# Tile sizes, first-tile attention, attend product, PSUM layout and engine loops of a chunked-attention and two-FFN kernel

## What is computed

```python
# q, k, v: (4, 8, 768, 64); mem_k, mem_v: (4, 8, 8, 64)
for c in range(768 // 32):               # chunks of 32 queries
    keys = [8 memory keys, 16 left, 32 own, 8 right]   # clipped at both ends
    scores = q_c @ keys.T / sqrt(64)
    a = exp(scores - max); a = a / (sum(a) + 1e-9)
    out[c] = a @ values
x  = out as (3072 tokens, 512)
x2 = (s * relu(x @ w_in1)**2 + b) @ w_out1           # 512 -> 2048 -> 512
h  = x2 @ w_in2;  result = (h * sigmoid(1.702 * h)) @ w_out2
```

## Time and profile before

| | us |
|---|---|
| median of 3 runs | 1269.33 |
| lowest and highest | 1268.78, 1270.19 |
| span of the profiled execution | 1269.2 |
| PE busy | 1252.3 |
| DVE, ACT, POOL busy | 655.9, 552.9, 96.9 |

### The profile page before, as it was taken

How to read it: one execution, slowest core, us unless ns; L and a number is a source line. 1 busy time by engine, 2 the same in 40 slices (tenths; PEclk the granted TensorE clock), 3 DMA queues, 4 the chain that set the end, 5 groups by cost and what they waited for, 6 DMA issues and landing times.

```text
span 1269.2 us, 20951 instructions
## 1 busy us (share of the span) xinstructions
PE 1252.3 (99%) x7168; PEld 1142.9 (90%) x7168; DVE 655.9 (52%) x2111; ACT 552.9 (44%) x1676; POOL 96.9 (8%) x78
## 2 busy tenths in 40 slices
PE   7999999999999999999999999999999999999998
PEld 5699999998999999999999999999999999999997
DVE  7788766666666666666645532333333332333322
ACT  7767555554555555555535532322222222222222
POOL 2255000000000000000005710000000000000000
PEclk9999999999999999999999999999999999999999
DMA  6545211212121212112013410000000101010000
GB/s 123 129 106 131 66 29 32 63 24 49 49 47 24 71 24 63 33 27 68 10 58 117 133 59 25 25 26 26 25 25 0 50 0 50 0 50 0 5 20 25
DMA packets 119555, 59.91 MB, mean 47 GB/s; under 512 B 93863, under 2 KB 110247, under 8 KB 119463
## 3 DMA queue, kind: packets, MB, share of 16 engines
q1 hardware_dynamic: 119463, 58.74, 17.6%
HBM read 46.14 MB, written 12.58 MB: 46 GB/s over the span
## 4 chain that ended last, share of the span: by engine, by line
PE 97%; DVE 2%; ACT 1%; issue 1%; DMA 0%; SPq 0%
PE psum L448 43%; PE psum L466 21%; PE psum L463 21%; PE psum L415 5%; PE psum L431 3%; PE psum L401 2%; PE psum L391 1%; PE psum L390 1%; DVE qk_lo L640 1%; ACT qk_hi L504 1%; DVE probs_n L671 0%; DVE masked L654 0%; DMA kv_raw<-in_mem_k_dram 0%; DVE x_lo L680 0%; DVE total_e L662 0%
## 5 line engine op out<-in xcount | busy, mean ns | idle before, releaser
L448 PE MATMUL psum<-x_hi,win_hi 128*128 128x384 f32 x1024 | 355.2, 347 | 0.0
L448 PE MATMUL psum<-x_hi,win_lo 128*128 128x384 f32 x1024 | 345.7, 338 | 0.0
L448 PE MATMUL psum<-x_lo,win_hi 128*128 128x384 f32 x1024 | 344.9, 337 | 0.0
L448 PEld LDWEIGHTS psum<-x_lo,win_hi 128*128 128x128 f32 x1024 | 193.2, 189 | 5.5
L448 PEld LDWEIGHTS psum<-x_hi,win_hi 128*128 128x128 f32 x1024 | 192.8, 188 | 5.6
L448 PEld LDWEIGHTS psum<-x_hi,win_lo 128*128 128x128 f32 x1024 | 192.7, 188 | 0.0
L466 PE MATMUL psum<-g_hi,wout_hi 128*128 128x384 f32 x512 | 171.6, 335 | 0.0
L466 PE MATMUL psum<-g_lo,wout_hi 128*128 128x384 f32 x512 | 171.5, 335 | 0.0
L466 PE MATMUL psum<-g_hi,wout_lo 128*128 128x384 f32 x512 | 171.3, 335 | 0.0
L640 DVE TENSOR_TENSOR qk_lo<-psum,qk_hi 64x128 fp32r<-64x128 f32 (+1 forms) x384 | 94.9, 275 | 128.0 <-ACT qk_hi L504 125.9
L539 ACT ACTIVATE g_hi<-gated 128x384 fp32r<-128x384 f32 x128 | 67.2, 525 | 196.5 <-PE psum L463 195.9
(11 more groups left out here) (61 smaller groups left out, 1585.6 us busy)
## 6 DMA issues: line engine op xcount, KB each, us to landing
w_raw<-in_moe_w_in_dram SPq DMA_DIRECT2D x32, 256.0 KB, 2.8
w_raw<-in_moe_w_out_dram SPq DMA_DIRECT2D x32, 256.0 KB, 2.8
kv_raw<-in_v_dram SPq DMA_DIRECT2D x32, 240.0 KB
kv_raw<-in_k_dram SPq DMA_DIRECT2D x31, 240.0 KB
x_scratch<-result SPq DMA_DIRECT2D x8, 768.0 KB, 3.3
kv_raw<-x_scratch SPq DMA_DIRECT2D x8, 768.0 KB, 4.3
q_raw<-in_q_dram SPq DMA_DIRECT2D x31, 192.0 KB
out_dram<-result SPq DMA_DIRECT2D x7, 768.0 KB, 3.6
```

Source lines behind the costliest of these rows:

```text
L448: last = nc.tensor.matmul(dst, w[:, f, kt, :], x[:, slot, kt, :], start=(i == 0), stop=(i == len(terms) - 1))
```

## The change

1. Part 0 is cut into tiles of 288, 288, 384, 384, 384, 384, 480 and 480 tokens; part 1 stays at 8 times 384.
2. Only 12 units (the first 288 tokens) come ahead of the first product, in 6 rounds of four heads each, with their own buffers and banks (`first_*` functions). Here the scores are 64-row products of 128 columns, POOL normalizes, and DVE copies the transposed probabilities. Three more rounds finish them and begin the next units.
3. `attend` takes v and the transposed probabilities, both split in hi and lo, and makes three fp32r passes with 128 weight columns and 192 moving columns for both heads at once. Half of the 128 x 192 result (the other head's values) isn't read. POOL splits v once for four units (`split_v`), ACT and DVE split the probabilities.
4. PSUM banks have one use in each phase: in steady state bank 6 holds transposed q/k and probabilities, bank 7 scores and attend result.
5. The units are spread evenly over the steps of a tile (`groups`): two groups of instructions for each unit, half a unit apart, put between single matmuls. 13 slots fall to tile 0, 16 to tiles 1 to 4, 20 to tiles 5 and 6. DVE takes its part of a group 6 or 4 matmul places later.
6. From unit 24 on POOL normalizes the probabilities; before that DVE does. In tile 0 DVE writes the hi of the w_in slices. x2 is loaded in pieces of one row block; `gated` has one buffer.
7. There are no engine loops; every instruction is written out.

In the core of the diff below stand, in this order: the loops that go, the tile table and the slots, waits of SP's loads of `w_in` slice 3 and `w_out` slice 1, POOL's order of work, the first scores and the attend on PE, the groups on PE and on DVE, PE's order ahead of the first product, and DVE's w_in copy in tile 0. `HALVES` is 6, `LEAD` 4, `FIRST` 12, `HP` 4, `QT` 96.

```diff
-            tile(mm=None, att=(0, 0, 0, True), refill=(0, 0, EARLY, 0, (NF - 3) // (EARLY - 1)))
-            tile(mm=0, part=0, slot=0, att=(1, 1, 0, True), refill=(0, EARLY, NF, 0, 1))
-            with eng.Fori(0, (NTILE - 4) // 2) as i:
...
+TILES = ((288, 288, 384, 384, 384, 384, 480, 480), (384,) * 8)
+AFTER = {1: 6, 2: 4}
+def beats_of(mm):
+    if mm >= M0 - 1:
+        return []
+    last = first_unit(mm + 2) if mm + 2 < M0 else UNITS
+    return list(range(FIRST - 1 if mm == 0 else first_unit(mm + 1), last))
...
+def pool_normalizes(n):
+    return n >= first_unit(2)
...
+                elif f == EARLY + 1:
+                    sp.wait_ge(s_attended, HALVES)
...
+                elif f == 1:
+                    sp.wait_ge(s_attended, HALVES)
...
+            for i in range(HALVES - 1):
+                first_normalize(i)
+            split_w_in(0, 0)
+            first_normalize(HALVES - 1)
+            split_w_in(0, 1)
+            split_v(FIRST // HP)
+            split_w_out(0, 0)
...
+            def first_score(i):
+                for p in range(2):
+                    for t, (a, c) in enumerate(((hi, hi), (hi, lo), (lo, hi))):
+                        for e in range(2):
+                            rows = slice(e * D, (e + 1) * D)
+                            last = nc.tensor.matmul(s_bank_s[p][e][0:QT, 0:P], a[rows, p * 224:p * 224 + QT],
+                                                    c[rows, p * 224 + QT:p * 224 + QT + P], start=(t == 0), stop=(t == 2))
...
             def attend(mm, att, u0):
...
-                for h in range(2):
-                    last = nc.tensor.matmul(out_bank(mm, u)[h * D:(h + 1) * D, 0:QT], v_raw[:, j % 2, c0:c0 + D],
-                                            pT[:, u % 2, h, :], start=True, stop=True)
+                if there(n - 1):
+                    pe.wait_ge(x_ready, nth(n - 1))
+                if there(n + LEAD - 2):
+                    pe.wait_ge(max_ready, nth(n + LEAD - 2))
+                pe.wait_ge(pT_ready, nth(n))
+                for i, (a, c) in enumerate(((v_hi, pT_hi), (v_hi, pT_lo), (v_lo, pT_hi))):
+                    last = nc.tensor.matmul(bank_o, a[:, j % 2, hp * P:(hp + 1) * P], c[:, n % 2, :],
+                                            start=(i == 0), stop=(i == 2))
...
+            def group(kind, n):
+                if kind == 1:
+                    if there(n + 1):
+                        transpose_probs(n + 1)
+                    if there(n + LEAD):
+                        transpose_qk(n + LEAD)
+                else:
+                    if there(n):
+                        attend(n)
+                    if there(n + LEAD - 1):
+                        score(n + LEAD - 1)
...
+            def group(kind, n):
+                if kind == 1:
+                    if there(n + LEAD):
+                        split_qk_lo(n + LEAD)
+                    if there(n + 1):
+                        split_pT_lo(n + 1)
+                    if there(n + 2):
+                        invert(n + 2)
+                else:
+                    if there(n + LEAD - 1):
+                        mask_and_max(n + LEAD - 1)
+                    if there(n):
+                        split_x_lo(n)
...
+            for r in range(HALVES + 3):
+                if r < HALVES:
+                    first_score(r)
+                if 0 <= r - 2 < HALVES:
+                    first_attend(r - 2)
+                if r >= HALVES:
+                    group(1, FIRST - LEAD + r - HALVES)
+                    group(2, FIRST - LEAD + r - HALVES)
+                if r + 2 < HALVES:
+                    first_transpose(r + 2)
+                if 0 <= r - 1 < HALVES:
+                    first_transpose_probs(r - 1)
...
+                        if place == 3 and mm == 0 and f + 2 < NF:
+                            split_w_in_hi(f + 2)
```

## The result

The changed kernel takes 1256.01 us (median of 4 runs, 1254.91 to 1256.32) where the kernel before takes 1269.6: a ratio of 0.9891, 95% interval 0.988 to 0.9903, or 13.6 us. The forecast was 1251.0 us, in a range of 1237 to 1266.

A forecast was written before the change was run, and what follows sets the result against it. PE's stream was taken as the bound: 34 (start) + 1.9 + 1072.1 (products) + 126.4 (units) - 1.3 + 1 + 10 + 2 = 1246.1 us for PE's end. With 3.3 behind it 1249, rounded up to 1251; range 1237 to 1266.

The forecast's parts named there:

- if the start stays over 40 us: Sign that the prediction is wrong: the first product, forecast at 34 us (bounds 30 and 38), begins later than 40 us.
- Products at other widths: Product matmuls in tiles of 288 and 480: 0.133 and 0.216 us each, nothing gained or lost overall, bound +2 us.
- Attend: Attend on PE: three passes at 0.11 us, two extra waits around 64-column weights go, unit 1.24 to 1.09 us.
- rival (c): Attend's three narrow fp32r passes cost as plain fp32, up to 0.31 us each: slower, up to 1321 us; chance 0.12.
- The time before the first product: Six rounds of 3.5 us from 8 us, then 5 us: first product at 34 us, 17.4 earlier.
- some 6 us less the overlap: Ahead of the first product: the operations from exp to x_lo behind the last round's masks.
- Tile 0: First tile of part 0: 10 us lost to DVE (bounds 0 and 18), 1 us stall for weights (0 to 4).
- DVE becomes the bound: In tile 0 DVE needs 4.65 us a step against PE's 4.07, which costs 10 us over 16 steps.
- Tiles 1 and 5: Part 0, a unit each 4.2 to 4.4 us against a loop of about 3.6: 2 us added for lateness.
- Rival (b): The DVE-POOL port binds through part 0, slowing tiles 1 and 5: 1263 us; chance 0.17 together with a late start.
- The loop jump: PE's wait of 2.1 us at the engine loop's jump goes away.
- The 2 us of rounding up: 1249 us raised to 1251 for groups between single matmuls: a first-matmul wait perhaps twice a unit, 0.02 x 116.

## Why the prediction came out as it did

**In one sum.** The forecast 1251.0, + 6.5 for the start (40.5 for 34), - 3.3 for the time from there to PE's end (1210.4, where the terms with the rounding left 1251 - 3.3 - 34 = 1213.7), + 0.1 for the end behind PE, + 1.8 between span and time, is 1256.1. The profiled execution took 1256.06. The range holds it. But the prediction's own list of signs says that it is wrong "if the start stays over 40 us", and the start is 40.5: that step failed, and other terms made up for part of it.

**Products at other widths: right.** 0.1327 us at 288 and 0.2166 at 480, for 0.133 and 0.216.

**Attend: right, mechanism and size.** Passes at 0.09 to 0.11 for 0.11, unit 5.2525 - 4.188 = 1.065 for 1.09. That is 0.025 x 116 = 2.9 us better than the sum. It makes rival (c) void, and the return to the old form shows both extra waits as its doing, though not that both come from its 64 columns. Of the two prices that the Trainium skill ("TensorE: Matmul & The Clock Gate") gave for a pass in the prediction, that of the weight load (107 ns) is nearer to the mean spacing of 102 ns than that of the columns (82).

**The time before the first product: the wrong step.** The rounds came as worked out, the last masks at 26.14 us for about 25.5, though PE waited 2.5 us in the second round for a load that I had not counted. What failed is the end of the term, "some 6 us less the overlap" behind the last masks. From the last masks to the first product it measured 14.4 us instead of 8.5. I had the added groups' split and masks in it, and left out that the first beat of tile 0, at place 0, puts unit 12's transposed probabilities ahead of the first product: guard, inversion and normalize of one more unit in a row, one of them held by POOL. The run with that group nine places later takes 3.7 of the 6.5 us away, and half of this was worth nothing to the time. Of the rest 0.6 is the later last mask. The other 2.2 lie in the three added rounds, where the chain runs without a gap through attend, the transposes of q and k and their splits on ACT and DVE (28.9 to 37.0 us), for which and for the last round's tail the term had left 5 us behind the sixth round.

**Tile 0: right in size, half right in mechanism.** I forecast 11 us lost (10 for DVE, 1 for weights); 12.7 were, and 2.6 at the lower clock for the 1.9 forecast. The cause, POOL's subtractions against DVE, is shown: with memsets in their place 10.5 us go, and 9.9 with POOL as busy as before. But the 0.81 us that I charged to the gate alone is 0.39, and as much again lies on copy, normalize and guard: 11.1 / 14 = 0.8 for a weight slice in all. "DVE becomes the bound" agrees with the chain, which lies on DVE for 40.5 of 71 us, but not with a sum of DVE's work alone: DVE is busy for 87%, and with 8 us moved from it to ACT tile 0 is no shorter, since ACT is then late. What PE waits for is the row of small operations on DVE from the sums to the transposes. PE shows no wait for weights, so the 1 us is put down to the same chain.

**Tiles 1 and 5: no loss.** 2 us were forecast; tile 1 takes 68.5 us where 51.0 + 16 x 1.065 = 68.0 would do, tile 5 88.27 for 67.0 + 20 x 1.065 = 88.3. Rival (b) isn't seen, since PE waits for POOL's normalize only 0.2 us in all from 117 to 620 us. The run with normalize on DVE shows the other side: with DVE's own normalize beside POOL's v_lo, 5.4 us are lost in the same tiles.

**The loop jump: right,** 2.1 us forecast, 2.0 measured alone. **The 2 us of rounding up** for insertions were not needed.

**Span and time.** I took the span as the time because it agreed with the median to 0.2 us. In every execution here that has both, of the kernel before too, the time is 1.7 to 2.0 us above the span, 1.8 nearly always (1256.06 and 1254.3 here). The execution profiled before must then have taken about 1271.0, 1.4 us over the median of 1269.6. That is why the step at PE's end, from 1265.86 to 1250.93 or 14.9 us, is 13.6 in the medians, and why the 1.8 us between span and time didn't show: that slow execution's span happened to equal the median.

**What the change is worth, part by part.** Attend's form gains 15.2 us (PE's end with and without), the loops 2.0, and the tile sizes cost 8.5. If parts add, some 6 us of the 14.9 are left for the new rounds of the first units, the placing of the groups and the banks, which were not run apart.

## What to carry to other kernels

When PE is the bound, look at the spacing ahead of and behind an odd matmul, not only at its own length: here three fp32r passes were as long as the two plain fp32 matmuls that they replaced and still gave 0.144 us back each time, because the matmuls around them came closer. Before an operation is shrunk so that it no longer covers others (a narrower first tile), write out the whole chain of small operations from one PE instruction to the next, with each operation's price beside a reading POOL, and include whatever stands ahead of the first matmul. A gain ahead of a stretch that another chain limits can be lost in that stretch, here half of 3.7 us in one run and all of 2.6 in another: test it there before adding it up. And when work is moved from a loaded engine, look at what the chain then runs through: the engine that took it may hold the same wait.

## What the hardware showed that I had not expected

- An operation on 96 x 2 elements, 0.155 us where POOL is idle, took 1.17 us (mean 432 ns in tile 0), held by a POOL subtraction of 1.26 us: the length of a DVE operation says nothing of what it can lose.
- Gate and normalize run at full speed beside POOL memsets (516 and 421 ns with POOL busy 53.4 of 66 us). The copy to fp32r and the guard don't (up to 0.75 us for 0.42, and up to 0.52 for 0.155).
- fp32r with 192 moving columns and 128 weight columns nearly keeps its rate: 0.10 us a pass in the mean, where 0.091 would be in proportion to the wider ones and plain fp32 takes 0.32 us for the 192 columns in its form with 64 weight columns.
